# Attention and gated product on one core: the mask and the pooling of v move to TensorE in the first four pairs, probability copies to ScalarE

## The reference

```python
q_d = q.reshape(B, H, 144, 4, D).mean(axis=3)      # the same for k and v
out_up = np.repeat(sm_attn(q_d, k_d, v_d), 4, axis=2)   # pooled attention, repeated
mask = np.abs(pos[:, None] - pos[None, :]) < 4          # band attention
scores = np.where(mask, scale * q @ k.T, -1e9)
out_local = softmax(scores) @ v
x = (out_up + out_local) as (2304 tokens, 512)
h = x @ w_in                                            # 512 x 2048
g = h * np.tanh(softplus(h))
out = g @ w_out                                         # 2048 x 512
```

## Time and profile before

| | us |
|---|---|
| median of 3 runs | 518.39 (517.86 to 518.90) |
| the profiled execution, its own time | 518.92 |
| span of that execution | 517.1 |
| TensorE busy in the span | 489.0 (95%) |
| VectorE busy | 242.2 (47%) |
| ScalarE busy | 170.8 (33%) |
| GpSimd busy | 129.5 (25%) |

### The profile page before, as it was taken

How to read it: one execution, slowest core, us unless ns; L and a number is a source line. 1 busy time by engine, 2 the same in 40 slices (tenths; PEclk the granted TensorE clock), 3 DMA queues, 4 the chain that set the end, 5 groups by cost and what they waited for, 6 DMA issues and landing times.

```text
span 517.1 us, 9118 instructions
## 1 busy us (share of the span) xinstructions
PE 489.0 (95%) x3748; PEld 437.2 (85%) x3748; DVE 242.2 (47%) x483; ACT 170.8 (33%) x362; POOL 129.5 (25%) x164
## 2 busy tenths in 40 slices
PE   6756999999999999999999999999999999999995
PEld 6645888988999998888888888889899998999994
DVE  4996698977322224275464455635322222122220
ACT  1355564655121114353453444434121111211111
POOL 4885556644100001151332413312000000000000
PEclk9867799999999999999999999999999999999999
DMA  8980831121010001122031140310010000100001
GB/s 252 325 305 5 310 96 48 48 97 27 23 61 1 0 1 48 74 85 83 14 96 50 49 146 13 96 49 0 1 63 0 2 0 1 41 22 0 1 0 61
DMA packets 15641, 33.58 MB, mean 65 GB/s; under 512 B 1776, under 2 KB 1904, under 8 KB 15600
## 3 DMA queue, kind: packets, MB, share of 16 engines
q1 hardware_dynamic: 15600, 33.00, 19.8%
HBM read 28.28 MB, written 4.72 MB: 64 GB/s over the span
## 4 chain that ended last, share of the span: by engine, by line
PE 88%; DVE 7%; issue 2%; ACT 1%; POOL 0%; DMA 0%; DVEq 0%; ACTq 0%
PE hidden L504 38%; PE acc L518 38%; PE att L410 2%; PE att L423 2%; PE att L479 1%; PE att L464 1%; PE acc L487 1%; PE att L445 1%; PE att L435 1%; DVE prob L587 1%; DVE small L592 1%; DVE prob L594 1%; DVE small L613 1%; DVE small L601 1%; PE att L472 0%
## 5 line engine op out<-in xcount | busy, mean ns | idle before, releaser
L504 PE MATMUL hidden<-x_high,w_in_high 128*128 128x384 f32 x384 | 131.0, 341 | 2.1 <-DVE x_odd L648 2.1
L504 PE MATMUL hidden<-x_high,w_in_low 128*128 128x384 f32 x384 | 130.5, 340 | 0.0
L504 PE MATMUL hidden<-x_low,w_in_high 128*128 128x384 f32 x384 | 129.8, 338 | 0.0
L790 ACT ACTIVATE g_full<-hidden 128x384 f32<-128x384 f32 x96 | 47.2, 492 | 243.0 <-PE hidden L504 242.9
L662 DVE CAST g_high<-g_full 128x384 fp32r<-128x384 f32 x96 | 38.5, 401 | 189.7 <-PE acc L518 144.5
L518 PE MATMUL acc<-w_out_high,g_high 128*128 128x512 f32 x288 | 115.1, 400 | 0.0
L518 PE MATMUL acc<-w_out_low,g_high 128*128 128x512 f32 x288 | 113.3, 393 | 0.0
L518 PE MATMUL acc<-w_out_high,g_low 128*128 128x512 f32 x288 | 113.3, 393 | 0.0
L504 PEld LDWEIGHTS hidden<-x_high,w_in_high 128*128 128x128 f32 x384 | 73.0, 190 | 6.5 <-DVE x_odd L648 2.5
L504 PEld LDWEIGHTS hidden<-x_low,w_in_high 128*128 128x128 f32 x384 | 72.9, 190 | 3.4
L504 PEld LDWEIGHTS hidden<-x_high,w_in_low 128*128 128x128 f32 x384 | 72.7, 189 | 0.0
(11 more groups left out here) (78 smaller groups left out, 469.8 us busy)
## 6 DMA issues: line engine op xcount, KB each, us to landing
v_win<-in_v_win SPq DMA_DIRECT2D x16, 320.0 KB
q_t<-in_q SPq DMA_DIRECT2D x16, 296.0 KB, 3.0
k_t<-in_k SPq DMA_DIRECT2D x16, 296.0 KB, 3.7
v_in<-in_v SPq DMA_DIRECT2D x16, 288.0 KB
out<-stage SPq DMA_DIRECT2D x18, 256.0 KB, 2.1
w_in_raw<-in_w_in SPq DMA_DIRECT2D x16, 256.0 KB, 11.3
w_out_raw<-in_w_out SPq DMA_DIRECT2D x16, 256.0 KB, 6.3
const<-in_const SPq DMA_DIRECT2D x1, 224.0 KB, 3.9
```

The costliest lines, as they stand in the source:

```text
L504: last = nc.tensor.matmul(hidden[:, g % HB, 0:TB], w, x[:, k, cols], start=(k == 0 and i == 0), stop=(k == KT - 1 and i == 2))
L790: nc.scalar.activation(g_full[:, g % 2], hidden[:, g % HB, 0:TB], ACT.Mish).then_inc(mish_ready, 1)
```

## The change

- `band_scores` of pairs 0 to 3 begins with an identity matmul of the mask into each of the two score banks (float32r copies of both, made once by ScalarE), and the score matmuls add to it. `band_maxima` of these pairs reduces PSUM directly and subtracts from PSUM into SBUF.
- `outputs` of pairs 0 to 3 multiplies with v's four token phases in turn, so 16 pooled matmuls stand for 4, and `pool_v` of these pairs is gone. For all pairs the loop over the heads becomes the outer one.
- `copy_probs` goes from VectorE; ScalarE's `copy_rest` makes all.
- x of pair 3 is rounded and split in two token pieces, 0 to 383 and 384 to 575; the first only needs `main_combined`.
- The queues are written out anew. Scoring of pair 4 comes behind the first three k-tiles of first products 0 and 1, whose fourth k-tiles follow. The slots of pairs 4 to 7 are now in half steps (before or behind a first product). Five w_in tiles are prepared ahead, and two of w_out; the initial `keep_busy` calls are 10 and 4 for 16 and 10.

```diff
+EARLY_IN = 5
+EARLY_OUT = 3
+ROUNDED_OUT = 2
+FIRST = 384
-WARM_UP = 16
-BUSY = 10
+WARM_UP = 10
+BUSY = 4
+def halves(n):
+    if n < 2 * HP:
+        return ((None, 9, 10), (12, 16, 17), (19, 23, 24), (26, 30, 31))[n - HP]
+    at = 2 * FT * (n // HP) + 8 * (n % HP)
+    return at - 1, at + 3, at + 5
...
+                    by_pe = n < AHEAD
+                    if by_pe:
+                        for h in range(2):
+                            nc.tensor.matmul(att[:, h, 0:T * WK], ident_r[:], mask_r[:], start=True, stop=False)
...
-                                    start=True, stop=True)
+                                    start=not by_pe, stop=not by_pe or t == T - 1)
...
-                    for kh in range(2):
-                        for h in range(2):
-                            last = nc.tensor.matmul(
-                                b[D * h:D * (h + 1), 1, OUT_POOL].rearrange("p (t g) -> p t g", g=GQ),
-                                s["v_pool"][:, kh, D * h:D * (h + 1)],
-                                s["prob_pool_t"][:, kh, :, h], start=(kh == 0), stop=(kh == 1))
+                    pooled = [(s["v_pool"], 0)]
+                    if n < AHEAD:
+                        pooled = [(inp(n)[2], r) for r in range(POOL)]
+                    for h in range(2):
+                        for kh in range(2):
+                            for i, (v, r) in enumerate(pooled):
+                                rows = v[:, kh, r, D * h:D * (h + 1)] if n < AHEAD else v[:, kh, D * h:D * (h + 1)]
+                                last = nc.tensor.matmul(
+                                    b[D * h:D * (h + 1), 1, OUT_POOL].rearrange("p (t g) -> p t g", g=GQ),
+                                    rows, s["prob_pool_t"][:, kh, :, h],
+                                    start=(kh == 0 and i == 0), stop=(kh == 1 and i == len(pooled) - 1))
...
+                for f in range(HB):
+                    first_product(0, f, range(KT - 1))
+                band_scores(AHEAD)
+                pooled_scores(AHEAD)
...
+                        burst(2 * g)
+                        first_product(j, f, range(KT - 1, KT) if g < HB else range(KT))
...
+                    if n < AHEAD:
+                        scores = att[:, 0:2, 0:T * WK].rearrange("p h (t k) -> p h t k", k=WK)
+                        nc.vector.tensor_reduce(top, scores, AX_X, ALU.max).then_inc(band_top, 1)
...
+                            last = nc.vector.tensor_tensor(
+                                x[:, windows].rearrange("p (h t) k -> p h t k", h=2), scores[:, :, lo:hi],
+                                top[:, :, lo:hi].rearrange("p h (t o) -> p h t o", o=1).broadcast_to(
+                                    [P, 2, hi - lo, WK]), ALU.subtract)
...
+                    if n == AHEAD - 1:
+                        act.wait_ge(main_combined, n + 1)
+                        nc.scalar.copy(x_high[:, k, 0:FIRST], x_of(n)[:, 0:FIRST]).then_inc(x_rounded, 1)
+                        act.wait_ge(combined, n + 1)
+                        nc.scalar.copy(x_high[:, k, FIRST:S], x_of(n)[:, FIRST:S]).then_inc(x_rounded, 1)
```

ScalarE's new queue in the lead-in, of which the prediction speaks:

```diff
                 band_exp(1)
+                copy_band(0)
                 pooled_exp(1)
-                copy_band(0)
                 copy_rest(0)
+                round_in(0)
                 band_exp(2)
                 pooled_exp(2)
                 upsample(0)
                 copy_band(1)
+                copy_rest(1)
                 round_x(0)
...
+                upsample(1)
+                round_x(1)
                 copy_band(2)
+                copy_rest(2)
                 round_in(2)
-                copy_rest(2)
-                round_x(1)
+                round_in(3)
                 upsample(2)
+                round_in(4)
                 copy_band(3)
+                copy_rest(3)
                 round_x(2)
```

More of the change, by code:

```diff
@@ L134, in program @@
         x_odd = over("x_odd", [P, S], 0)
+        mask_r = over("mask_r", [P, T * WK], 0, F32R)
+        ident_r = over("ident_r", [P, P], 1, F32R)
         for s in sets:
@@ L274, in _ @@
                 sp.wait_ge(out_ready, AHEAD)
-                for f in range(EARLY, 7):
+                for f in range(EARLY_OUT, 6):
                     load_w_out(f)
                 load_qk(AHEAD + 1)
-                for f in range(7, FT):
+                for f in range(6, FT):
                     if f == 13:
-                        sp.wait_ge(x_split, AHEAD)
+                        sp.wait_ge(x_split, split(AHEAD - 1))
                     load_w_out(f)
@@ L487, in keep_busy, with first_product @@
                         nc.tensor.matmul(acc[:, 2, 0:P], zeros, zeros, start=True, stop=True)
-                def first_product(j, f):
+                def first_product(j, f, tiles=range(KT)):
                     g = FT * j + f
-                    if g == 0:
-                        pe.wait_ge(combined, AHEAD)
+                    if g == 0 and tiles[0] == 0:
+                        pe.wait_ge(combined, AHEAD - 1)
                     if g >= HB:
@@ L498, in first_product @@
                     cols = slice(at, at + TB)
-                    for k in range(KT):
-                        if f == 0:
-                            pe.wait_ge(x_split, HP * (0, 1, 1, 2, 3, 3)[j] + k + 1)
+                    for k in tiles:
+                        if j == 0 and k == KT - 1:
+                            pe.wait_ge(x_split, AHEAD)
+                        elif f == 0:
+                            pe.wait_ge(x_split, split(HP * (0, 1, 1, 2, 3, 3)[j] + k))
                         high, low = w_in_high[:, f, P * k:P * (k + 1)], w_in_low[:, f, P * k:P * (k + 1)]
@@ L505, in first_product @@
                                                     start=(k == 0 and i == 0), stop=(k == KT - 1 and i == 2))
-                    last.then_inc(hidden_ready, 1)
+                    if tiles[-1] == KT - 1:
+                        last.then_inc(hidden_ready, 1)
                 def second_product(j, f):
                     g = FT * j + f
+                    if g == 0:
+                        pe.wait_ge(combined, AHEAD)
                     if j == 0:
@@ L533, in _ @@
                 pooled_scores(2)
+                outputs(0)
                 band_scores(3)
-                outputs(0)
                 turn_band(1)
@@ L653, in split_x @@
                     k, cols = ring(n)
-                    dve.wait_ge(x_rounded, n + 1)
-                    nc.vector.tensor_tensor(x_low[:, k, cols], x_of(n), x_high[:, k, cols].bitcast(F32),
-                                            ALU.subtract).then_inc(x_split, 1)
+                    x = x_of(n)
+                    for lo, hi in ((0, FIRST), (FIRST, S)) if n == AHEAD - 1 else ((0, S),):
+                        dve.wait_ge(x_rounded, split(n) - (hi < S))
+                        to = slice(cols.start + lo, cols.start + hi)
+                        nc.vector.tensor_tensor(x_low[:, k, to], x[:, lo:hi], x_high[:, k, to].bitcast(F32),
+                                                ALU.subtract).then_inc(x_split, 1)
                 def split_g(g):
@@ L800, in _ @@
                 act.preload_act_table_set(EXP_TABLES)
+                act.wait_ge(const_loaded, 16)
+                nc.scalar.copy(mask_r[:], mask).then_inc(const_rounded, 1)
+                nc.scalar.copy(ident_r[:], ident).then_inc(const_rounded, 1)
                 band_exp(0)
```

239 lines of the change are left out of this document (122 added, 117 removed).

## The result

The changed kernel is slower: 530.88 us (528.82 to 532.02, 4 runs) against 518.59 (517.86 to 518.90) for the kernel before in the same series, a ratio of 1.0235 with an interval of 1.0201 to 1.0268. The forecast was 510.8 with a range of 506.3 to 521.0. The profiled execution took 530.69 us, its span 528.9.

What follows compares the result with a forecast made beforehand. The lead-in was taken as bound by chains between engines, the body by TensorE. -9.5 + 1.6 - 1.2 + 0.7 + 0.8 = -7.6 us from 518.9 gave 511.3, 510.8 on the median's scale; range 506.3 to 521.

Steps and rivals of the forecast that it cites:

- Mask on TensorE: Lead-in, pairs 0 to 3: VectorE saves 0.8 us a pair, and another 1.4 at each of two slow subtractions.
- Four token phases of v: Pooled outputs of pairs 0 to 3: 32 instructions take 1.95 us a pair, 3.9 if TensorE doesn't look ahead.
- rival 3: Phases serial in the lead-in only: 3.9 us a pair, +7.2, time 518.0, no change; chance 0.13.
- rival 4: Head order serial everywhere: +7.2 in the lead-in, +4.4 in twelve later bursts, 522.4 us; chance 0.18.
- Half clock: Lead-in: TensorE's clock falling after new holes before outputs(2) and outputs(3), allowed 1.7 us.
- Rival 5: Lead-in set by ScalarE's copies (2 us more) or lasting half clock (+2 + 1.2): 513 to 515; chance 0.12.
- The sum of the lead-in: TensorE reaches the first product at 43.0 us instead of 52.5: -9.5.
- scores(4) behind the first k-tiles: Start of the products: pair 4's scores, formerly hidden in the lead-in, cost TensorE 1.6 us: +1.6.
- the clock at its start: First 24 product instructions: 2.5 us lost to half clock, half of it regained: -1.2, bounds -2.5 and 0.
- Body: Token blocks after the lead-in: +0.7 for ScalarE's copies, +0.8 for new slots of pairs 4 to 7, head order 0.
- the copies: Body: a copy of 0.37 us net moves to ScalarE and TensorE waits for it in two blocks: +0.7.
- the head order from pair 4 on: Later bursts, pairs 4 to 15: four instructions a head, overtaking three: 0, bound +4.4 us.

Runs made afterwards that it cites:

- before_mask: Kernel before with only the mask's products on TensorE, the new maxima and the earlier start: 515.24 us, ratio 0.9947.
- busy_holes: Changed kernel with 12 and 6 zero products in TensorE's waits in front of outputs(2) and outputs(3): 521.84 us, ratio 1.0077.
- inner_busy: Changed kernel with the heads alternating in the pooled products, plus 14 and 8 zero products in front of outputs(2) and outputs(3): 517.07 us, ratio 0.9991.
- scores4_back: Changed kernel with pair 4 scored and exponentiated in the lead-in again and pairs 4 to 7 on their old slots: 514.65 us, ratio 0.9936.
- squeezed: scores4_back with the changed kernel's slots for pairs 5 to 7: 514.71 us, ratio 0.9939.

## Why the prediction was wrong

The forecast was -7.6 and +11.8 came, 19.4 apart in the profiled span: 10.75 of it in the lead-in, 7.0 in block 1 (8.17 where +1.2 was forecast) and 1.7 behind it (2.36 for +0.7). Going through its own steps:

- *Mask on TensorE*: right. outputs(0) started at 18.83 (predicted 18.5), no slow subtraction was left, and before_mask shows the step alone (with the shorter start that belongs to it) at 3.2 us of lead-in.
- *Four token phases of v*: wrong, the step that failed first. "I take 1.95" rested on a reach of 16 matmuls; the band rows showed a reach of three and no more, and the prediction said so itself. 3.70 was measured where the bound was 3.9, so rival 3's mechanism is what happened, and rival 4's further cost in the later bursts did not come: with four instructions to a head a reach of three suffices, and the later bursts kept their 0.7 us (0.72 in eleven of the twelve, 0.71 before; the other, at 77.73, took 0.90 with the clock falling to 0.50 at 78.13). It costs 3.9 us of lead-in at full clock (busy_holes against inner_busy).
- *Half clock*: wrong in size, 7.65 instead of 1.7. I priced it by the length of the new waits. What decided was what TensorE did afterwards: 13 us of pooled products, nearly all at 0.50 and twice as long. Rival 5 had the mechanism ("half clock stays through outputs(2), (3) and the first products") and a third of the price (2 on top of the 1.7).
- *The sum of the lead-in*: right but for these two. 43.0 forecast, 53.78 measured: +3.9 for the order, +7.65 - 1.7 for the clock, +0.9 for what inner_busy still has over 41.3; together 10.75.
- *scores(4) behind the first k-tiles*: wrong, and the largest single miss: block 1 grew by 8.2 instead of +1.6 - 1.2 + 0.8. I counted TensorE's 1.6 us and looked at nothing else of the step. Of the -1.2 for the clock at its start some 0.7 came: 3.9 us at 0.50 behind the first product instead of 5.3. Behind the scores come pair 4's exponentials, for which ScalarE leaves the gate's table and returns (64.12 and 67.25, 1.28 us each), its normalization on GpSimd, and beside this and two weight splits there a split of g on VectorE that takes 3.64 us, where the quickest near it take 0.56; the gate at 73.97 waits for that split, the copies for the gate, and outputs(4) 2.3 us for the copies. Of the 7.9 us by which the two windows differ, 4.1 are TensorE's idle time (5.2 in the block, 1.1 before) and 3.8 its longer busy time (87.56 against 83.78), in which are the scores, 1.6, and the half clock from 78.1 to 81.5, after the wait of 2.3, 1.5 (12 products in 3.64 us, 2.13 at full clock); with the 0.7 that the start gained, some 1.4 us of the busy time stay unassigned. That moving pair 4 here causes all of it is shown (scores4_back, squeezed). How it falls between the table loads, the slow split and what stands behind them was not separated, but the slow split as such is not new. The kernel before has one in its first token block too, and scores4_back another (3.64 at 72.79), and behind neither does TensorE wait for the gate or for the copies; in the kernel after the gate and pair 4's copies stand behind the slow split. The kernel before, VectorE:

```profile
77.41 3.63 DVE L664 TENSOR_TENSOR g_low<-g_full,g_high 128x384 fp32r<-128x384 f32 x1
```

- *Body*: the copies +0.7, as forecast; another 1.5 by the clock's fall in block 3. The slots of pairs 5 to 7: 0 (at unlike clocks), the head order from pair 4 on: 0, x in two pieces: 0, all within the forecast or its bounds.

The range ended at 521.0 because each rival moved one term. Here two of them and an unpriced third went together.

## What to carry to other kernels

Let small matmuls that are to share the array alternate in the program between the parts of the array: the same 32 instructions took 2.18 us so and 3.70 in two long runs, since only three waiting instructions were passed here. Price a wait of TensorE by the work behind it at the clock that it may leave, 0.50 here, not by its own length, and keep a case in which the clock doesn't fall: it did in two of three profiles of the same lead-in. A few zero products in the waits gave back 7.65 us here, more than the mask's part brought. Work that is moved behind another stage takes its helpers along: follow its exponentials, tables and normalization on their engines before pricing TensorE's part.

## What the runs showed of the hardware that was not expected

- TensorE started a pooled instruction beside others on the other column half when three instructions were waiting ahead of it, not when more were (27.8, 20.7 and 15.4 steps of 0.1225 us for the three orders).
- Being busy did not bring the clock back here: 0.50 from 37.2 to 57.7 us with TensorE busy 20.0 of the 21 us from 36 to 57. What ran until 53.78 was mostly 72 by 64 products; with 12 zero products of the full array in front of outputs(2), and 6 in front of outputs(3), the same products ran at 1.00, in 3.70 us.
- A VectorE subtraction of two SBUF operands, 128 by 384, took 3.64 us while GpSimd normalized and split weights (below), those at 66.30 and 74.79 took 0.56. The 68 VectorE operations that write the tile `prob` with one operand in PSUM (`att`) took 0.69 us at most each, in the kernel before and after alike.

GpSimd's timeline beside that subtraction (70.24 to 73.88):

```profile
68.73 1.26 POOL L361 TENSOR_TENSOR prob<-prob,small 128x640 f32<-128x640 f32 x1 [3.75 <-DVE small L669]
69.95 1.02 POOL L369 TENSOR_TENSOR prob_pool<-prob_pool,small 96x432 f32<-96x432 f32 x1
70.94 2.52 POOL L375 TENSOR_TENSOR w_in_low<-w_in_raw,w_in_high 128x512 fp32r<-128x512 f32 x2
```
